# Attention and two channel mixers on one core: batches between products, norm steps spread over pairs, low halves on GpSimd, and a held first load order

## The reference, cut to what matters

```
B, H, S, D = 2, 8, 768, 64;  block, window = 32, 16;  d_model = H * D = 512
attention: k_sum = max, v_sum = mean of each 32 keys / values
           softmax over (|i - j| < 16 keys) and (24 block maxima + log 32)
           out = a @ concat(v, v_sum)
x  = attention out as [B, S, 512]
u  = x + (relu(x^T @ w_tok1) @ w_tok2)^T             # w_tok1 768x256
x2 = u + relu(u @ w_ch1) @ w_ch2                     # 512 -> 1536 -> 512
xn = (x2 - mean) / sqrt(var + 1e-6) * g_ln
out = x2 + relu(xn @ w2_ch1) @ w2_ch2                # 512 -> 2048 -> 512
```

## Time and profile before

| what | value |
|---|---|
| median of 3 runs (lowest to highest) | 664.21 us (663.83 to 666.57) |
| the profiled execution, its own time | 664.86 us |
| its span, first to last instruction | 663.1 us |
| TensorE busy | 598.0 us, 90% of the span |
| VectorE, ScalarE, GpSimd busy | 359.4, 244.9, 247.2 us |
| mean granted TensorE clock | 0.964 of full speed |
| DMA, first 110 us | 130 to 238 GB/s |

### The profile page before, as it was taken

One profiled execution on the slowest core, in us unless ns is written; L12 is line 12 of the kernel. 1 busy time (PEld: TensorE's weight loads), 2 busy tenths in 40 slices (PEclk: granted clock), 3 DMA queues, 4 the chain that ended last, 5 costly groups with the idle time before them and its releaser, 6 DMA issues.

```text
span 663.1 us, 8253 instructions
## 1 busy us (share of the span) xinstructions
PE 598.0 (90%) x2976; PEld 513.7 (77%) x2976; DVE 359.4 (54%) x695; ACT 244.9 (37%) x450; POOL 247.2 (37%) x247
## 2 busy tenths in 40 slices
PE   5999998878999899986998798699998999999997
PEld 2777887757888787875787687588887788898896
DVE  5568656283444558654442876523445784444435
ACT  3577655242332235332323532233332633333321
POOL 5464744170333663320334533332227433333300
PEclk9899999898999989988999799889998999999999
DMA  8887540001111011111101111101111111111302
GB/s 230 238 232 217 162 130 2 1 0 64 63 65 63 2 63 64 64 63 64 63 20 46 64 63 64 63 1 64 64 64 63 65 63 65 64 64 63 128 0 96
DMA packets 24896, 50.34 MB, mean 76 GB/s; under 512 B 7596, under 2 KB 7832, under 8 KB 24856
## 3 DMA queue, kind: packets, MB, share of 16 engines
q1 hardware_dynamic: 24304, 49.37, 22.6%
q10 hardware_dynamic: 552, 0.44, 0.3%
HBM read 46.07 MB, written 3.15 MB: 74 GB/s over the span
## 4 chain that ended last, share of the span: by engine, by line
PE 65%; DVE 18%; ACT 8%; issue 5%; POOL 1%; DMA 1%; SPq 0%; DVEq 0%; ACTq 0%; POOLq 0%
PE bank L478 63%; DVE down_w L880 5%; DVE hidden L955 3%; ACT hidden L796 3%; DVE in_t L880 3%; ACT down_w L792 2%; DVE c_raw L1022 2%; DVE c_raw L1028 1%; PE bank L571 1%; DVE c_raw L1036 1%; DVE neg_scores L898 1%; DVE to_turn L993 1%; DMA k_sb<-k_w 1%; ACT probs L723 1%; PE bank L513 1%
## 5 line engine op out<-in xcount | busy, mean ns | idle before, releaser
L478 PE MATMUL bank<-down_w,hidden 128*128 128x512 f32 x1008 | 272.2, 403 | 3.4 <-DVE hidden L955 3.3
L478 PEld LDWEIGHTS bank<-down_w,hidden 128*128 128x128 f32 x1008 | 191.5, 193 | 34.5 <-issue 5.4
L478 PE MATMUL bank<-in_t,up_odd 128*128 128x384 f32 x588 | 124.5, 348 | 10.4 <-DVE c_raw L1022 4.3
L478 PE MATMUL bank<-in_t,up_even 128*128 128x384 f32 x588 | 122.1, 345 | 12.4 <-ACT p L802 5.5
L478 PEld LDWEIGHTS bank<-in_t,up_odd 128*128 128x128 f32 x588 | 108.8, 195 | 22.5 <-issue 9.6
L478 PEld LDWEIGHTS bank<-in_t,up_even 128*128 128x128 f32 x588 | 107.8, 194 | 23.1 <-ACT p L802 6.7
L796 ACT ACTIVATE hidden<-c_raw 128x384 fp32r<-128x384 f32 x84 | 44.2, 527 | 216.6 <-DVE c_raw L1022 118.2
L420 POOL TENSOR_TENSOR up_even<-sums_up,up_even 128x1024 fp32r<-128x1024 f32 x14 | 33.5, 2396 | 158.8 <-ACT up_even L786 158.7
L420 POOL TENSOR_TENSOR up_odd<-sums_up,up_odd 128x1024 fp32r<-128x1024 f32 x14 | 33.6, 2400 | 145.5 <-ACT up_odd L786 145.5
L955 DVE SCALAR_TENSOR_TENSOR hidden<-c_raw,hidden 128x384 fp32r<-128x384 f32 x84 | 59.0, 702 | 48.0 <-ACT hidden L796 48.0
L1003 DVE TENSOR_TENSOR u<-bank,p 128x384 f32<-128x384 f32 x28 | 15.6, 557 | 69.5 <-PE bank L478 68.0
(11 more groups left out here) (87 smaller groups left out, 724.2 us busy)
## 6 DMA issues: line engine op xcount, KB each, us to landing
raw_up<-w_ch SPq DMA_DIRECT2D x28, 512.0 KB, 4.3
raw_down<-w_ch SPq DMA_DIRECT2D x28, 512.0 KB, 3.5
k_sb<-k_w SPq DMA_DIRECT2D x16, 273.0 KB, 4.3
v_own<-v_w SPq DMA_DIRECT2D x8, 390.0 KB, 3.3
q_sb<-q_t SPq DMA_DIRECT2D x8, 384.0 KB, 5.4
v_turned<-v_t SPq DMA_DIRECT2D x8, 384.0 KB, 3.4
out<-natural SPq DMA_DIRECT2D x12, 256.0 KB, 3.1
tok_stage<-w_tok SPq DMA_DIRECT2D x4, 384.0 KB, 3.9
```

Of the source, the lines that this page charges most:

```text
L478: return nc.tensor.matmul(dst, lhs, rhs, start=start, stop=stop, skip_group_check=True)
```

## The change

**Opening.** The first load is now that of the turned values, then keys, queries and values of pair 0; then SyncE waits until the first means have landed in `v_far` (`sp.wait_ge(ld_mean[0], 32)`) before it issues any load of pairs 1 and 2. The sum of pair 0's values is one VectorE reduction in place of the GpSimd tree; the means are sent from ScalarE's queue; the mask comes in two pieces; TensorE turns the sums ahead of the first scores, with 6 further warm matmuls behind the copy.

**First pair.** The token mixer's six last output tiles (`last_mix`) stand between the products of pair 0; turned batches 2 to 7 of batch 1 come earlier; of each group's seven inputs VectorE makes only two low halves and GpSimd the other five.

**Pairs.** `BATCHES_AT` moves batches by a pair or so; down units now also stand behind each batch; `low_down` comes behind c_raw 1; `sum_inputs` of groups 2 and 3 comes a pair earlier.

**Norm.** bn_stats of a tile follows its `add_out`; moments, square root, scales and the six rows all stand in `j` = 1.

**Memory.** The order of the tiles in SBUF changes, `pad` shrinks from 640 to 16.

```
-BATCHES_AT = ((2, 2, 2, 2, 0, 0), (0, 0, 2, 3, 3, 0), (0, 0, 2, 2, 2, 2, 0, 0), (0,) * 8)
-T_AT = (4, 5, 6)
-DOWNS_AFTER = (2, 2, 2, 2, 1, 1, 2)
+DOWNS_AFTER = {0: (2, 2, 2, 2, 1, 1, 2), 2: (2, 2, 1, 1, 1, 1, 1, 1, 2), 3: (2, 1, 1, 1, 1, 1, 1, 1, 1, 2)}
+BATCHES_AT = ((0, 2, 2, 2, 2, 0), (0, 0, 3, 3, 2, 0), (0, 0, 2, 2, 2, 2, 0, 0), (0,) * 8)
+T_AT = (4, 4, 5)
+DVE_IN = 2
...
 SyncE
-            load_k(0)
-            load_q(0)
             load_turned(0)
+            load_k(0)
+            load_q(0)
             load_v(0)
+            sp.wait_ge(ld_mean[0], 32)
             load_turned(1)
             load_k(1)
             load_q(1)
-            send_means(0)
             load_v(1)
...
 ScalarE
-            act.dma_start(mask_sb[:], mask).then_inc(ld_mask, 16)
             act.dma_start(ident[:], identity).then_inc(ld_ident, 16)
+            act.dma_start(mask_sb[:, 0:2], mask[:, 0:2]).then_inc(ld_mask, 16)
+            copy_means(0, mix_bank[0:NSUM, mean_at])
+            send_means(act, 0)
+            act.dma_start(mask_sb[:, 2], mask[:, 2]).then_inc(ld_mask_end, 16)
...
 GpSimd
+            def low_input(g, i):
+                pool.wait_ge(in_high, 7 * g + i + 1)
+                src = t_in[:, T_OF[i]] if i in T_OF else raw_block(i)
+                nc.gpsimd.tensor_tensor(in_t[:, i, 1], src, in_t[:, i, 0].bitcast(F32), ALU.subtract
+                                        ).then_inc(in_low_pool, 1)
+                pool.wait_ge(in_low_pool, (7 - DVE_IN) * g + i - DVE_IN + 1)
...
             for q in range(1, NQ):
                 g, j = group_of(q)
+                if j == 0:
+                    for i in range(LATE_IN, 7):
+                        low_input(g, i)
                 if q + 1 < NQ:
                     sum_weights(q + 1)
                     low_sums(q + 1)
...
+                if g + 1 < NGROUP and j == PAIRS_OF[g] - 1:
+                    for i in range(DVE_IN, LATE_IN):
+                        low_input(g + 1, i)
...
 VectorE, pair(q)
+                if scaling:
+                    row_stats(g - 1, 4)
+                    row_stats(g - 1, 5)
...
+                if scaling:
+                    row_moments(g - 1)
...
+                if scaling:
+                    row_scales(g - 1)
...
                 nc.vector.tensor_tensor(c_raw[:, 1], product_bank(q, 5)[:, 0:HN], u3[:], ALU.add).then_inc(c_made, 1)
-                if ending:
-                    low_input(g + 1, 2)
-                    low_input(g + 1, 3)
+                low_down(q)
                 low_hidden(q, 2, c_raw[:, 1])
```

More of the change, by code:

```diff
@@ L44 @@
 KB = 3
-PAD = 640
+PAD = 16
 AHEAD = 3
@@ L255, in batch_bank, with send_means @@
             return up_bank[(7 * q + 7 + k - 8) % 2]
+        def send_means(queue, r):
+            i = r % 2
+            queue.wait_ge(mean_copied, r + 1)
+            if r >= 2:
+                queue.wait_ge(pv_done, NT * (r - 1))
+            else:
+                queue.wait_ge(far_init, r + 1)
+            for h in range(2):
+                at = SUM_ROW[h]
+                queue.dma_start(v_far[at:at + NSUM, i, :, 1 + h * D:1 + (h + 1) * D],
+                                v_mean[:, i, h * D:(h + 1) * D].rearrange("p (t n) -> p t n", t=1)
+                                .broadcast_to([NSUM, NT, D])).then_inc(ld_mean[i], 16)
         block = ctx.enter_context(nc.Block())
@@ L586, in _ @@
             pe.wait_ge(warm_ready, 1)
-            for _ in range(WARM):
+            for _ in range(WARM[0]):
                 mm(mix_bank[:], warm[:, 0:P], warm[:], True, True)
-            pe.wait_ge(k_clear, CLEARS)
+            pe.wait_ge(ld_ident, 16)
+            pe.wait_ge(init_done, 3)
+            turn_sums(0, mix_bank[:, mean_at])
+            pe.wait_ge(mean_copied, 1)
+            for _ in range(WARM[1]):
+                mm(mix_bank[:], warm[:, 0:P], warm[:], True, True)
             scores(0)
@@ L660, in down, with last_mix @@
                     last.then_inc(down_done, 1)
+            def last_mix(t):
+                if t == 0:
+                    pe.wait_ge(x_done, 2 * NPAIR)
+                    pe.wait_ge(h_low, 4)
+                if t >= 2:
+                    pe.wait_ge(u_done, NT + t - 1)
+                for m in range(2):
+                    mix_out(t, m, o_bank[t % 2])
             def pair(q):
@@ L666, in pair @@
                 units = iter(UNITS)
+                after = DOWNS_AFTER[BATCHES_AT[g][j]]
                 for i in range(7):
@@ L690, in pair @@
                     up(q, i)
+                    if q == 0 and i < NT:
+                        last_mix(i)
                     if q:
-                        for _ in range(DOWNS_AFTER[i]):
+                        for _ in range(after[i]):
                             down(q - 1, *next(units))
                 for b in range(BATCHES_AT[g][j]):
-                    if g and turned % 8 == 0 and b == 0:
-                        pe.wait_ge(nat_ready, NT * g)
+                    if turned % 8 == 0 and b == 0:
+                        if g:
+                            pe.wait_ge(nat_ready, NT * g)
+                        else:
+                            pe.wait_ge(u_done, 2 * NT)
                     if b < 2:
@@ L701, in pair @@
                     turn_batch(turned + b)
+                    for _ in range(after[7 + b]):
+                        down(q - 1, *next(units))
             for q in range(NQ):
@@ L863, in _ @@
             high_x(2 * NPAIR - 1)
-            copy_batch(1)
+            for k in range(1, 4):
+                copy_batch(k)
+            high_input(0, 0)
             for m in range(2):
+                copy_batch(4 + 2 * m)
                 high_h(1, m, score_bank[1 - m])
-                copy_batch(2 + m)
-            high_input(0, 0)
-            for k in range(4, 8):
-                copy_batch(k)
-            for i in range(1, 7):
+                copy_batch(5 + 2 * m)
+                if m == 0:
+                    high_input(0, 1)
+            for i in range(2, 7):
                 high_input(0, i)
@@ L1000, in pair @@
                 opening = g > 0 and j == 0
+                normed_group = g in (1, 2)
+                scaling = normed_group and j == 1
+                if q == 0:
+                    add_mixed(1, 0, o_bank[0])
                 dve.wait_ge(up_done, 7 * q + 2)
@@ L1003, in pair @@
                 nc.vector.tensor_tensor(u2[:], product_bank(q, 1)[:, 0:HN], p1[:], ALU.add).then_inc(u_made, 1)
-                if opening:
-                    for i in range(LATE_IN, 7):
-                        low_input(g, i)
+                if q == 0:
+                    add_mixed(1, 1, o_bank[1])
+                if scaling:
+                    row_stats(g - 1, 4)
+                    row_stats(g - 1, 5)
                 if q and q + 1 < NQ:
@@ L1087, in _ @@
                 low_h(1, m, score_bank[1 - m])
-            for t in range(NT):
-                add_mixed(1, t, o_bank[t % 2])
-                if t >= 2:
-                    low_input(0, t - 2)
-            for i in range(4, 7):
+            for i in range(DVE_IN):
                 low_input(0, i)
```

164 lines of the change are left out of this document (93 added, 71 removed).

## The result

| | before | changed |
|---|---|---|
| median of runs | 664.27 us | 645.13 us (644.37 to 646.50, 4 runs) |
| ratio, 95% interval | | 0.9707 (0.9680 to 0.9735): faster |
| profiled execution / its span | 664.86 / 663.1 us | 646.50 / 644.7 us |
| TensorE busy / idle | 598.0 / 65.1 us | 597.3 / 47.4 us |
| mean granted clock | 0.964 | 0.958 |

A forecast was written before the change was run, and what follows sets the result against it. TensorE's waits and the half speed after them bound the kernel. Terms 1.0 + 0 + 9.3 + 18.7 + 16.8 - 0.5 sum to 45.3 us off 664.86, giving about 619 us, range 608 to 634.

The forecast's parts named there:

- Bounds and yardstick: Whole kernel: TensorE's waits, each followed by some us at half speed, cost time; a pair without waits takes 15.84 us.
- Term 4, the norm: Groups 1, 2: norm done in `j` = 1 ends waits of 2.10 and 5.56 us; whole term gains 18.7 and 16.8.
- Term 4, the new wait: First pair of groups 1 to 3: ScalarE waits for GpSimd's weight sums, delaying TensorE; 5.0 us in groups 1, 2.
- Term 3: Group 0, pairs 1 to 5: down units around batches remove waits; 82.6 us in place of 91.91, 9.3 gained.
- Term 2: Pair 0: output tiles fill waits, wait moves to `p`, copied at 145.5 to 148.5; no gain, bounds 4 us.
- Term 1: Opening and attention: first value product 3.0 us earlier, about 14.1, mostly lost again through held loads; 1.0 us gained.
- Term 5: Last group: wait about 1.5 us more than pair 20 had, last down units about 1.0 earlier; loss of 0.5.
- GpSimd is the bound at each group change: Group changes: low halves take 2.46 or more, VectorE's steps slow too, wait doubles; about 633 us, chance 0.16.
- GpSimd keeps up: GpSimd's low halves all take 1.85, no new wait, first pair wins 1 to 2 us; about 607, chance 0.15.
- The norm is not where it is said to be in time: VectorE overflows in `j` = 0 and 1, batches of pairs 8 and 14 wait; about 640, 0.07 shared with starved loads.
- the clock does not hold: From pair 1 on, granted clock falls below 0.90 with TensorE always busy; above 665 us, 0.05 with other losses.
- The hold starves attention: Attention: each pair's loads trail by 3 us for eight pairs; about 643 us, 0.07 shared with the norm's lateness.

The follow-up runs named there:

- (6): Changed kernel with the norm's stats, moments, square root, scales and rows back where they stood before: 658.2 us, ratio 0.9893.
- (1): Changed kernel with GpSimd's weight sums ahead of the three late low halves in the first pair of a group: 628.16 us, ratio 0.9448.
- (9): Repaired kernels: changed kernel with edits (1), (3), (4), input 1's cast later: 605.37 us with SyncE's hold, 605.80 without, 605.99 without and low halves on VectorE replacing (1).
- (3): Changed kernel with the four `t_in` steps moved to the last pair of the group, between weight sums and their low half: 629.51 us, ratio 0.9465.
- (8): Changed kernel with `low_down` back in front of c_raw 1, except in pair 0: 654.92 us, ratio 0.9851.
- (7): Changed kernel with all down units of a pair ahead of its batches, as before the change: 647.34 us, ratio 0.9728.
- 5: Two kernels: changed kernel without SyncE's wait for the first means, 643.79 us; changed kernel with the whole opening of before, 643.92 us.
- (4): Changed kernel with ScalarE copying `p` ahead of four of its input casts in pair 0: 637.5 us, ratio 0.9566.

## Why the prediction was wrong, point by point

- **Bounds and yardstick: right.** Pairs without waits take 15.72 to 15.84, and what was to be won was TensorE's waits and the half speed after them; the repaired kernels win both. Of the prediction's own signs of being wrong one came, the clock of group 1 at 0.94, below the 0.95 named; and two signs of being right did not, for TensorE idles 7.4 us in group 1, not under 5, and 3.06 in pair 4, not under 1.
- **Term 4, the norm: right.** Pairs 8 and 14 lose their waits; undoing this part alone costs 12.4 us (6), 18.8 in these two pairs less 4.6 elsewhere.
- **Term 4, the new wait: right in place, in chain and nearly in size.** "3.2 in all, and some 1.8 at half speed: 5.0" at a group change; removed (1), it gives 5.2 and 5.7 in groups 1 and 2. In pair 6 TensorE waited 2.72 + 0.32 and then ran 5 us at half speed, into pair 7, about 2.6 lost and not 1.8. There is some luck in the 3.2: VectorE's steps were taken at their own lengths, and 1.9 of the 2.72 us are a `hidden` held by GpSimd. Groups 1 and 2 are 8.2 and 7.2 short of the forecast mainly by the next point; and pairs 7 and 13 take 17.5, not 15.84, even in the kernel with all repairs and the hold (9).
- **Term 3: the failed step.** "c_raw 2 and the copy of the batch each have 0.7 us or more of other work ahead of them". That does not hold where `t_in` runs beside VectorE's steps: there c_raw 2 came 3.06, 3.07 and 2.96 us late, in pairs 4, 10 and 17, which cost 16.1 us (3), 15.1 by the pairs. Of the 26.9 us between the 45.3 forecast and the 18.4 gained this is more than half. It was missed in group 0, and in groups 1 and 2 too, where term 4 uses the same ends of pairs. It could have been seen: the change's own table (`T_AT`) puts `t_in` into the pair with the last batches, and the earlier trace rows already show 2.46 for a `t_in` beside VectorE. I had priced that contention for GpSimd's side only, though the trace of before has VectorE's side too, a `hidden` of 2.24 and a `down_w` of 2.86 in pair 4. No batch stood behind them there, but c_raw 1 did, and TensorE waited 1.9 us for it at the start of pair 5. The credit was incomplete as well: the gain in pairs 1 to 3, which is real (16.4), comes from `low_down` behind c_raw 1 (8) at least as much as from the down units between batches (7).
- **Term 2: right in its mechanism.** `p` was copied at 147.91 (forecast 145.5 to 148.5) and TensorE waited 5.99 for it; pair 1 starts at 161.86, 0.9 beyond the forecast's 158 to 161. From the end of the wait to pair 1 it takes 13.4 us, where 10.9 and 1.5 for half speed were forecast: clock 0.82 in that stage, 0.92 before. In the other kernels whose pair 0 was not edited pair 1 starts between 158.6 and 163.2, so the miss of terms 1 and 2 is no larger than the scatter of the opening.
- **Term 1: first product 14.13 (forecast 14.1)**, a hit with luck in it, for the same opening gave 13.88 to 16.04 in other profiles. VectorE came to the keys of pair 1 at 17.89, not at 16. The -1.3 can't be told from the +1.0, nor either from zero (5, 9).
- **Term 5:** -4.1 in place of -0.5, the same wait as in term 4: pairs 20 and 21 fall from 18.7 to 16.4 and 16.6 when the sums go first. It cost 4.4 us and was priced at 1.5.
- **Rivals.** The nearest was "GpSimd is the bound at each group change", 633: VectorE's own steps are held up, which was its ground. The run shows that it still had only the group changes and not the pairs with `t_in`. "GpSimd keeps up" (607) did not come, nor did "The norm is not where it is said to be in time", "the clock does not hold" and "The hold starves attention": no `to_turn`, no stage after 161.86 below 0.94, attention within 1.3 us. That the clock holds with TensorE always busy is shown by the repaired kernel: 1.00 over 440 us of work.

## What to carry to other kernels

Offloading an elementwise step from VectorE to GpSimd is not priced by its own length: ask which two-SBUF-input steps of VectorE will start while it runs, add to those what is then left of the GpSimd step, and see what stands behind them in VectorE's list. Where nothing urgent stood behind them here, it cost nothing measurable: the repaired kernels with the low halves on GpSimd and on VectorE are equal (9). In an in-order queue, put what another engine waits for (the weight sums) ahead of what is wanted late; here the order of two calls was worth 17 us and the move to another engine nothing. And price a wait of TensorE of 2 to 3 us at more than its length, for the half speed that follows: here 9.1 us of waits gave back 15 to 16, and 8.0 us of idle time at the group changes 15.3. The short ones are another matter: after the wait of 1.65 us in (4) six down matmuls took 1.62, full speed.
